# A top-k attention and expert kernel: thresholds tested for six tiles at a time in a ring of 18, masks started one group of tiles sooner, and the order of one DMA queue rewritten

## The reference

```python
B, H, S, D = 2, 8, 576, 64           # q, k, v
scores = scale * np.matmul(q, k.transpose(0, 1, 3, 2))
kth = np.partition(scores, -32, axis=-1)[..., -32:-31]
scores = np.where(scores >= kth, scores, -1e9)
attn = np.exp(scores - scores.max(-1, keepdims=True))
attn = attn / (attn.sum(-1, keepdims=True) + 1e-9)
x = np.matmul(attn, v)               # rearranged to 1152 tokens x 512
# router: expert_idx = argmax(x @ w_gate), gate_w = its softmax value
# each expert takes at most capacity = 288 tokens, in order of the tokens
h = np.maximum(np.einsum('ecd,edf->ecf', disp, w1), 0.0)   # F = 1024
y = np.einsum('ecf,efd->ecd', h, w2)
out[i] = gate_w[i] * y[expert_idx[i], pos[i]]
```

## Time and profile before

| What | us |
|---|---|
| median of three runs | 468.13 |
| the profiled execution | 468.17 |
| its span, first to last instruction | 466.4 |
| outside the span | 1.8 |
| DVE busy between 20 and 260 | 230 |
| PE begins to work on masks of the first tile | 72 |
| last DVE search of the attention ends | 266 |
| last PV ends, experts' phase begins | 292 |

### The profile page before, as it was taken

One profiled execution on the slowest core, in us unless ns is written; L12 is line 12 of the kernel. 1 busy time (PEld: TensorE's weight loads), 2 busy tenths in 40 slices (PEclk: granted clock), 3 DMA queues, 4 the chain that ended last, 5 costly groups with the idle time before them and its releaser, 6 DMA issues. The chain is left out here.

```text
span 466.4 us, 8667 instructions
## 1 busy us (share of the span) xinstructions
PE 424.5 (91%) x2753; PEld 348.8 (75%) x2753; DVE 285.9 (61%) x1393; ACT 241.8 (52%) x428; POOL 239.7 (51%) x229
## 2 busy tenths in 40 slices
PE   2986768989899899899899999999999999999993
PEld 1653336767687777687788888786999999999771
DVE  2599799999999999999899853501011122021210
ACT  2233358888878878798688894032312121222320
POOL 4054459889888798898899675031001010120310
PEclk9999999999989999999899999999999999999998
DMA  4220205024041134021200105759999785867500
GB/s 101 53 48 5 51 1 142 3 47 107 21 138 28 28 116 116 1 70 49 94 1 2 27 3 201 262 183 366 324 319 335 275 288 193 273 222 236 191 22 19
DMA packets 53538, 57.85 MB, mean 124 GB/s; under 512 B 34286, under 2 KB 34286, under 8 KB 53488
## 3 DMA queue, kind: packets, MB, share of 16 engines
q1 hardware_dynamic: 51344, 52.51, 36.5%
q0 software_dynamic: 2144, 4.73, 2.8%
HBM read 45.39 MB, written 13.79 MB: 127 GB/s over the span
## 5 line engine op out<-in xcount | busy, mean ns | idle before, releaser
L471 POOL TENSOR_TENSOR rest<-below,scores 128x576 f32<-128x576 f32 x69 | 96.1, 1409 | 49.7 <-DVE below L1124 49.7
L656 PE MATMUL ps_o<-v_aug,pT 128*128 128x128 f32 (+5 forms) x800 | 118.2, 287 | 0.0
L656 PEld LDWEIGHTS ps_o<-v_aug,pT 128*128 128x128 f32 (+3 forms) x800 | 99.7, 183 | 13.4 <-issue 6.1
L476 POOL TENSOR_TENSOR probs<-scores,probs 128x576 f32<-128x576 f32 x72 | 101.0, 1418 | 2.8 <-ACT probs L948 2.8
L1059 DVE MAX8 cand<-scores 128x8 f32<-128x96 f32 x432 | 72.5, 243 | 13.8 <-ACT scores L922 13.8
L1025 ACT ACTIVATE scores<-ps_s 128x288 f32<-128x288 f32 x64 | 26.3, 411 | 104.0 <-PE ps_s L866 104.0
L922 ACT ACTIVATE scores<-ps_s 128x576 f32<-128x576 f32 x72 | 46.2, 648 | 44.2 <-PE ps_s L600 26.7
L866 PE MATMUL ps_s<-scores 128*128 128x192 f32 (+3 forms) x448 | 66.5, 306 | 0.0
L866 PEld LDWEIGHTS ps_s<-scores 128*128 128x128 f32 x448 | 64.4, 191 | 1.0 <-issue 0.7
L627 PE MATMUL ps_t<-ident,probs 128*128 128x128 f32 (+1 forms) x360 | 56.4, 289 | 8.8 <-issue 2.4
L539 POOL DMA_INDIRECT out_dram<-yo,numbers x15 | 13.7, 916 | 96.0 <-DVE yo L1358 94.5
(11 more groups left out here) (129 smaller groups left out, 397.7 us busy)
## 6 DMA issues: line engine op xcount, KB each, us to landing
w_sb<-in_moe_w_dram SPq DMA_DIRECT2D x9, 2048.0 KB, 13.2
scores<-in_moe_w_dram SPq DMA_DIRECT2D x7, 2048.0 KB, 10.3
dispatched<-empty SPq DMA_DIRECT2D x18, 257.0 KB, 4.1
scores<-dispatched SPq DMA_DIRECT2D x21, 192.8 KB, 3.5
out_dram<-empty SPq DMA_DIRECT2D x9, 256.0 KB, 2.8
q_nat<-in_q_dram SPq DMA_DIRECT2D x16, 128.0 KB, 2.3
k_nat<-in_k_dram SPq DMA_DIRECT2D x16, 128.0 KB, 2.4
v_aug<-in_v_dram SPq DMA_DIRECT2D x16, 128.0 KB, 2.4
```

The costliest lines, as they stand in the source:

```text
L471: nc.gpsimd.tensor_tensor(rest[:, n % 3, :], below[:, n % 3, :], score_tile(n), ALU.mult).then_inc(rest_ready, 1)
L476: nc.gpsimd.tensor_tensor(probs[:, n % PROBS, :], score_tile(n), probs[:, n % PROBS, :], ALU.subtract).then_inc(masked_ready, 1)
L656: last = nc.tensor.matmul(dst, lhs, v_aug[0:keys, g % 2, c, h, 0:width], start=(c == 0), stop=(c == TT - 1))
```

## The change

Five things are changed together.

- **Tests of six tiles.** Instead of one test for each of six pairs and then six tests of three tiles, eleven tests of six tiles and two of three: 13 tests for 12. Test i of six covers groups 2i and 2i + 1; DVE finds its flags at the end of group 2i + 2 and reads them in group m = 2i + 3, again after the second tile. Small buffers (`tops`, `next8`, `count`, `thr`, `edge`, `nmax`) become a ring of 18 places, indexed by the tile number.
- **Masks sooner.** `due` is 3(m - 2) where it was 3(m - 3), without the rule that took four or five a group at the end. So the first masks are made in group 3, not 4. Group 23 makes six, behind the next to last pick.
- **LEAD = 20**, was 22: every step of excess, T and PV moves two steps of s towards the scores.
- **`normalise`** of a pair comes one group sooner, in groups m = 7, 8, 10, 11 and so on to 22, 23. It is called 12 times in the loop, as before.
- **SP's list** has its 13 flags' DMAs in other places. The first, `gather_bad(0)`, stays where it was, behind `load_qk(3)`.

The diff, cut to its core:

```diff
-    LEAD = 22
+    LEAD = 20
-    PAIRWISE = PAIRS - 2
-    CHECKS = PAIRWISE + 3 * (PAIRS - PAIRWISE)
-    ENDING = 3 * PAIRWISE
+    SIXES = GROUPS // 2 - 1
+    CHECKS = SIXES + 2
+    SLOTS = 2 * TILES
...
         def ends_check(m):
 
-            return m % 3 == 2 or m >= ENDING
+            return m % 2 == 1 or m >= 2 * SIXES
...
             load_qk(2)
             load_qk(3)
             gather_bad(0)
...
             sp.wait_ge(empty_ready, 4)
+            gather_bad(1)
             load_qk(4)
             fill(0, 4)
-            gather_bad(1)
+            gather_bad(2)
             load_qk(5)
+            load_v(2)
             fill(4, 8)
-            gather_bad(2)
-            load_v(2)
+            gather_bad(3)
...
-                due = 3 * (m - 3) if m <= ENDING + 1 else min(4 * (m - ENDING) + 3 * ENDING - 9, ALL - 8)
+                due = 3 * (m - 2) if m < GROUPS - 1 else 6 * SIXES
...
-                if g >= 2 and tiles.start == 0:
-                    act.wait_ge(exp_ready, TILES * (g - 1))
+                if first >= SLOTS:
+                    act.wait_ge(exp_ready, first + n - SLOTS)
...
                     for i in range(CHECKS):
-                        if m == (3 * i + 4 if i < PAIRWISE else i - PAIRWISE + ENDING + 2):
+                        if m == (2 * i + 3 if i < SIXES else i + SIXES + 2):
                             if j == 1:
                                 counted = count_bad(i)
                             if j == 2:
...
-                if m >= 8 and m % 3 == 2 and m < GROUPS - 1:
-                    normalise(m // 3 - 2, 0)
-                if m >= 9 and m % 3 == 0 and m < GROUPS:
-                    normalise(m // 3 - 3, 1)
-                if m >= GROUPS - 2 and m < GROUPS:
-                    normalise(PAIRS - 3, m - GROUPS + 2)
+                if m >= 7 and m % 3 == 1 and m < GROUPS:
+                    normalise((m - 7) // 3, 0)
+                if m >= 8 and m % 3 == 2 and m < GROUPS:
+                    normalise((m - 8) // 3, 1)
```

More of the change, by code:

```diff
@@ L268, in check_of, with slots_of @@
         def check_of(n):
[L270 removed]
+            return n // 6 if n < 6 * SIXES else SIXES + n // 3 - 2 * SIXES
         def tiles_of(i):
[L274 removed]
+            return (6 * i, 6) if i < SIXES else (6 * SIXES + 3 * (i - SIXES), 3)
+        def slots_of(i):
+            first, n = tiles_of(i)
+            return slice(first % SLOTS, first % SLOTS + n)
         def ends_check(m):
[L278 removed]
+            return m % 2 == 1 or m >= 2 * SIXES
         def copies_until(e):
```

140 lines of the change are left out of this document (65 added, 75 removed).

## The result

| | before | after |
|---|---|---|
| median, us (all four runs) | 468.69 (467.48 to 469.70) | 484.45 (483.94 to 493.84) |
| the profiled execution | 468.17 | 484.19 |
| granted TensorE clock, mean | 0.988 | 0.973 |
| pick ahead of the last six masks | 257.42 | 273.17 |
| start of T(60) | 261.86 | 278.12 |

The changed kernel is slower: ratio 1.0334, 95% interval 1.0298 to 1.0369. I had forecast slower, at 477.4 with 474 to 481 around it. The direction is right, and the size is short by 6.8 us of 16.0 in the profiled executions.

A forecast was written before the change was run, and what follows sets the result against it. DVE's groups were taken to bound the time until about 256 us, PE's backlog the rest. DVE 9.9 us late puts T(60) 9.2 later; other terms 0: 468.2 + 9.2 = 477.4 us, range 474 to 481.

The forecast's parts named there:

- What bounds the kernel: Whole program: DVE's groups set the time until about 256 us, PE's backlog of 14 tiles the rest.
- DVE at the first test: Group 3: DVE waits 12.9 us for the first flags, so group 4 begins at 65.19, where group 5 did.
- DVE up to the last pick: From 65.19 to group 23: one more group, 9.10 us, and one more test read, 0.81, make DVE 9.9 us late.
- SP's other moves: SP's queue, flags' DMAs 2 to 12: they stand behind loads issued early enough, nothing waits, so 0.
- From T(60) on PE has the same work, and what feeds it is faster: PE's last stretch: no gaps from T(60) at 271.1, so the end moves by 9.2 us.
- Which tile PE waits for: PE after the last pick at 267.3: T(60) waits for mask 60 and starts at 271.1, 9.2 us later than before.
- router_ranks(0): Step 92, now behind PV(68): marks covered by 0.4 us, leading expert's weights by 5, both costed at nothing.
- The rival of the clock: PE's last stretch begins at the lower clock: 480.7 us if T(60) and T(61) run slow, 479.0 for one; 9%.
- the weights were not in the way of the scatter: Rival at the second batch's scatter: expert weights still loading delay it, costing 1 to 3 us, 478.5 to 480.5; 8%.
- Nothing was absorbed: Rival at PE's last stretch: its backlog of 14 tiles absorbs the late group and the end stays at 468; 4%.
- The early test costs nothing, and the kernel gets faster: Rival in group 3: first flags' DMA goes out when found, or PE's step 15 comes 13 us sooner; 465.5 us; 5%.

The follow-up runs named there:

- two experiments that take it away in different ways: The changed kernel with the first three transposes of x two tiles later, 480.28 us; the changed kernel with useless matmuls ahead of T(18) and T(54), 485.29 us.
- the kernel with both flags sooner: The changed kernel with the first flags' DMA ahead of pair 3's loads and the fourth's ahead of v loads and fills: 473.24 us, ratio 1.0063.

## Why the prediction was right and wrong

- **What bounds the kernel** (DVE's groups up to 256, PE's backlog after): right. The kernel before with a DVE that is 9.5 us late at the pick ends 10 us later, and the distance from placing to the experts is 15.84 in before and after alike.
- **DVE at the first test**, 12.9 us of wait and one group late: right to 0.1 us, by rows of the kernel before alone.
- **DVE up to the last pick**, 9.9 us: right for the work, and 5.9 short for the waits (273.17 for 267.3). "The DMA waits in the loop were 2.2 us" and "this term may lose 2.2 or gain about as much" was too narrow a bound: the second stall alone is 3.73, and DVE's waits for picks, which the sum does not have, are 3.0 more.
- **SP's other moves: "Nothing there waits, so: 0"**: this is the step that failed. In place of 0 the runs show a wait of 3.73 us at the fourth test, and about 6 us of time with what follows it. I had looked at whether each load comes soon enough for its user. I had not asked what stands ahead of each flags' DMA and what that waits for, which is the very question I put to the first one. The loads of pair 5 wait for step 33 of PE, 106.1 in the profile after, and with these eight issues and eight more ahead of it the flags' DMA cannot go before 115.9. The same question, asked for all 13, would have found it. With that one DMA moved the kernel takes 477.38 us, for 477.4 forecast (477.04 to 481.75 over its runs).
- **"From T(60) on PE has the same work, and what feeds it is faster"**, and LEAD as a change with no price: LEAD moves T, PV and the transposes of x against those of q and k. I checked the distance for `router_ranks(0)` and for nothing else in that step. It is 1.7 to 2 us in the changed kernel, by two experiments that take it away in different ways.
- **Which tile PE waits for** (T(60), 3.8 us behind the pick): the size came out with the stall gone (270.53 - 266.41 = 4.1), and the mechanism did not, so this is luck. "PE has done everything up to T(59) by then" is not so. In the kernel with the fourth flags sooner, where the clock does not hide it, PE waits last ahead of T(58) and has no idle time ahead of T(60):

```profile
264.31 0.74 PE L634 MATMUL ps_t<-ident,probs 128*128 128x128 f32 x5 [0.51 <-ACT pT L967]
...
269.74 0.86 PE L678 MATMUL ps_s<-ident,x 128*128 128x128 f32 x5
270.53 0.76 PE L634 MATMUL ps_t<-ident,probs 128*128 128x128 f32 x5
```

  From T(58) to T(60) are 6.2 us there and in the kernel before alike (255.65 to 261.86), and in the kernel before T(60) starts 4.4 us behind the pick. So mask 60 behind the pick, on which the term rests, is not what PE waits for. In the changed kernel it is 4.95 us, where PE itself is late.
- **router_ranks(0)** and the covers of the marks and of the leading weights: right, 0, and as thin as reckoned. PE does not wait for the marks with LEAD 20; with LEAD 19 it waits 1.71 us, and the time behind it grows by 2.0 and 6.4 (in the second partly at the lower clock).
- **The rival of the clock** was right as a mechanism and was held apart too cleanly. I gave it 9% as an alternative to the main case; it came on top of it. The Trainium skill (TensorE: Matmul & The Clock Gate, "HAM oscillation") says that a TensorE that waits between bursts starts the next burst cold; the trace after agrees, at 130 to 146 and at 258 to 269, with 2.64 us for a PV that takes 1.47. It does not do so behind every wait: behind 0.79 us at 106.91 the five transposes take 0.74. In the kernel with the fourth flags sooner the clock is down to 0.66 in 250 to 260 too, and the time is as forecast, for PE still waits for ACT behind it (0.51 us at 264.31). So what the lower clock costs is decided by what stands behind the slow instructions.
- **The other rivals**: the weights were not in the way of the scatter in the changed kernel (16.1 at placing, at the first and at the second matrix). Nothing was absorbed. "The early test costs nothing, and the kernel gets faster", in the form in which the flags' DMA goes out when they are found, is the kernel with both flags sooner: 473.2 against the 465.5 that I gave it. By the rows ACT and POOL are late there between 57 and 94 us; no kernel tries that part alone.

## What to carry to other kernels

When an operation stays in place in a queue while the work around it moves, follow it backwards: what stands ahead of it, and which other engine's step does that wait for. Ask this of every entry of the queue, not only of the first one; here two waits of loads for TensorE, passed on through SyncE to VectorE, were worth 11 of the 16 us with what followed from them, and the first of them in the kernel before still 3. A wait taken away is not a gain of its length: 12.96 us brought 4.1, and 3.73 us brought about 6, by what the other engines did behind it. A constant that shifts two loops against each other also shifts everything that is timed by either; list the steps in which they now meet.

## What the hardware showed that I had not expected

- A wait of 3.73 us on one engine went with about 6 us of the kernel's time. Part of the difference is TensorE's clock, which is 0.61 in the 10 us in which a wait of 2.65 ends, just ahead of its longest step; with the clock held there DVE gained 3.2 us up to 256 us.
- With 18 small matmuls in that wait the granted clock was 1.00 from 130 to 150 us (0.61 and 0.71 without).
- ACT started two instructions 1.1 and 1.5 us after all that the profile shows had been ready, in one of the two kernels that had matmuls added, and the first of them in the other too. The cause is open.
- The spread differs from kernel to kernel, and why is not shown: nine runs of the kernel before with its flags sooner lie within 2.9 us, and twelve of the changed one with both flags sooner and NEXT 4 within 7.7.
